# Reordering VectorE, ScalarE and GpSimd in the first and last steps of a dense layer behind attention and experts

## What is computed

```
def _moe_ref(x, w_gate, w1, w2):          # N=3072 tokens, D=512, E=8, F=1024
    ...
        h = np.maximum(xe @ w1[e], 0.0)
        ye = h @ w2[e]
        out[mask] = gate_w[mask, None] * ye

def _moe2_ref(x, w_in, w_out):            # w_in 512 x 2048, w_out 2048 x 512
    h = x @ w_in
    g = h - np.tanh(h)
    return (g @ w_out).astype(np.float32)
```

## Time and profile before

| | us |
|---|---|
| median of 3 runs | 1126.31 (1126.26 to 1127.74) |
| profiled execution, its own time | 1127.19 |
| its span | 1125.4 |
| PE busy | 1090.5 (97%) |
| DVE, ACT, POOL busy | 611.1, 478.8, 491.3 |

### The profile page before, as it was taken

One profiled execution on the slowest core, in us unless ns is written; L12 is line 12 of the kernel. 1 busy time (PEld: TensorE's weight loads), 2 busy tenths in 40 slices (PEclk: granted clock), 3 DMA queues, 4 the chain that ended last, 5 costly groups with the idle time before them and its releaser, 6 DMA issues.

```text
span 1125.4 us, 17079 instructions
## 1 busy us (share of the span) xinstructions
PE 1090.5 (97%) x5993; PEld 870.8 (77%) x5993; DVE 611.1 (54%) x1326; ACT 478.8 (43%) x1016; POOL 491.3 (44%) x494
## 2 busy tenths in 40 slices
PE   8999998799999999999989999999999999999995
PEld 5766765588888888888867888888888888888884
DVE  5787777232223222322258666666666666666664
ACT  6788875324233424351354333333333333333331
POOL 3246625617016345483175335335335335435432
PEclk9999999899999999999999999999999999999998
DMA  7545832534215243464241100001010010000000
GB/s 255 196 129 172 269 108 95 169 121 148 86 57 188 94 159 122 139 217 159 66 132 57 31 17 38 19 20 38 10 29 38 1 38 38 1 1 38 1 1 38
DMA packets 37916, 99.44 MB, mean 88 GB/s; under 512 B 8272, under 2 KB 8400, under 8 KB 32720
## 3 DMA queue, kind: packets, MB, share of 16 engines
q1 hardware_dynamic: 29392, 52.30, 15.0%
q0 software_dynamic: 8448, 46.17, 11.9%
HBM read 75.84 MB, written 22.61 MB: 87 GB/s over the span
## 4 chain that ended last, share of the span: by engine, by line
PE 88%; DVE 5%; POOL 3%; issue 2%; ACT 1%; DMA 1%; POOLq 0%; DVEq 0%; SPq 0%; ACTq 0%
PE bank L676 22%; PE bank L668 21%; PE bank L604 14%; PE bank L618 14%; PE bank L462 4%; PE bank L428 3%; PE bank L444 2%; PE bank L610 2%; DVE prob L932 1%; PE bank L591 1%; POOL weights L1299 1%; PE bank L656 1%; POOL sq L1389 1%; PE bank L504 1%; PE bank L494 1%
## 5 line engine op out<-in xcount | busy, mean ns | idle before, releaser
L1299 POOL TENSOR_TENSOR weights<-raw,weights 128x1024 fp32r<-128x1024 f32 x72 | 171.3, 2399 | 201.7 <-ACT weights L724 201.1
L668 PE MATMUL bank<-mT_hi,weights 128*128 128x512 f32 x768 | 252.2, 390 | 1.7 <-DVE mT_lo L1126 1.7
L676 PE MATMUL bank<-weights,gT_hi 128*128 128x512 f32 x768 | 242.7, 397 | 5.6 <-DVE gT_lo L1183 5.4
L1388 POOL TENSOR_SCALAR ser<-ser 128x512 f32<-128x512 f32 x96 | 63.8, 665 | 286.7 <-DVE ser L1165 286.6
L676 PEld LDWEIGHTS bank<-weights,gT_hi 128*128 128x128 f32 x768 | 142.7, 190 | 39.6 <-DVE gT_lo L1183 11.0
L668 PEld LDWEIGHTS bank<-mT_hi,weights 128*128 128x128 f32 x768 | 144.4, 188 | 32.0 <-DVE mT_lo L1126 2.0
L676 PE MATMUL bank<-weights,gT_lo 128*128 128x512 f32 x384 | 150.9, 393 | 0.0
L604 PE MATMUL bank<-weights,mT_hi 128*128 128x512 f32 x464 | 148.0, 400 | 1.5 <-issue 1.5
L668 PE MATMUL bank<-mT_lo,weights 128*128 128x512 f32 x384 | 149.5, 389 | 0.0
L618 PE MATMUL bank<-weights,hT_hi 128*128 128x512 f32 x464 | 148.7, 401 | 0.0
L875 ACT ACTIVATE bank<-bank 128x512 f32<-128x512 f32 x96 | 55.9, 582 | 213.9 <-DVE ser L1175 213.9
(11 more groups left out here) (141 smaller groups left out, 1577.8 us busy)
## 6 DMA issues: line engine op xcount, KB each, us to landing
raw<-w_all POOLq DMA_DIRECT2D x32, 1024.0 KB, 5.5
raw<-w_all SPq DMA_DIRECT2D x8, 1024.0 KB, 7.0
sorted_y<-ys SPq DMA_DIRECT2D x30, 257.0 KB, 3.3
xs<-sorted_x SPq DMA_DIRECT2D x29, 257.0 KB, 2.8
kT<-kt SPq DMA_DIRECT2D x24, 264.0 KB, 2.8
qT<-qt SPq DMA_DIRECT2D x24, 256.0 KB, 3.2
v_in<-vt SPq DMA_DIRECT2D x24, 256.0 KB, 3.8
raw<-sorted_y SPq DMA_DIRECT2D x20, 257.0 KB, 2.7
```

Of the source, the lines that this page charges most:

```text
L668: done = e.matmul(bank[HB[n % 3]][:, :], wt[:, f // 2, c, cols], x[:, c, :], start=(c == 0 and m == 0), stop=(c == CH - 1 and m == 2))
L676: done = e.matmul(bank[YB[i]][:, :], x[:, n % 3, rows], wt[:, f, :], start=(f == 0 and m == 0), stop=(f == GCH - 1 and m == 2))
L1299: e.tensor_tensor(lo, src, hi.bitcast(F32), ALU.subtract).then_inc(s_w_lo, 1)
L1388: e.tensor_scalar(row, row, SERIES_2, 1.0, ALU.mult, ALU.add).then_inc(s_ser, 1)
```

## The change

- **Last expert.** DVE splits low halves 6 and 7 of `w_in` after its (first) slot, on a new semaphore; GpSimd's steps 1 and 2 lose them, and the fourth load of `w_out` moves ahead of its step 0. PE waits on the new semaphore for these two.
- **First steps.** DVE's low half 0 of `w_out` goes ahead of series(0); the comparison of step 0 goes from GpSimd to DVE; in step 1 curve(0) comes first, then series(1), then g_lo(0). ScalarE's step 1 has square(1) and tanh(1) ahead of g_hi(0).
- **Steps 2 to 94.** DVE's g_lo(n-1) stands at the end of step n, behind low half n-1 of `w_out` where there is one; at the end of a group it now stands ahead of the two copies.
- **Last steps.** In step 95 DVE does curve(94) ahead of series(95), then g_lo(94), then the comparison of step 95. PE runs four more matmuls, whose result nobody reads, between down(94) and down(95).

```
 tensor:
                     if j == 0 and f % 2 == 0:
-                        e.wait_ge(s_w_lo, 8 * W_IN + f // 2 + 1)
+                        if f // 2 < 6:
+                            e.wait_ge(s_w_lo, 8 * W_IN + f // 2 + 1)
+                        else:
+                            e.wait_ge(s_in_lo, f // 2 - 5)
...
+                    if m == STEPS - 1:
+                        e.wait_ge(s_graw, m - 1)
+                        for _ in range(4):
+                            e.matmul(bank[HB[(m - 2) % 3]][:, :], gT_hi[:, (m - 1) % 3, 0:P], woh[:, 0, :],
+                                     start=True, stop=True)
 scalar:
+                if n < STEPS:
+                    square(n)
+                    tanh(n)
                 if n == 1:
                     e.wait_ge(s_row_ids, GROUP)
                     e.wait_ge(y_all, 1)
-                    g_hi(0)
-                    square(1)
-                    tanh(1)
-                else:
-                    if n < STEPS:
-                        square(n)
-                        tanh(n)
-                    if 2 <= n <= STEPS:
-                        g_hi(n - 1)
+                if 1 <= n <= STEPS:
+                    g_hi(n - 1)
 vector, experts:
                 slot_body()
+                if x == E - 1:
+                    for n, y in enumerate((6, 7)):
+                        src, hi, lo = w_half(W_IN, y)
+                        e.wait_ge(s_w_hi, 8 * W_IN + y + 1)
+                        e.tensor_tensor(lo, src, hi.bitcast(F32), ALU.subtract).then_inc(s_in_lo, 1)
 vector, second layer:
+            def small(n):
+                e.wait_ge(s_w, n + 1)
+                u = sq[:, n % 2, :]
+                e.tensor_scalar(u, u, SMALL_U, None, ALU.is_gt).then_inc(s_small_dve, 1)
...
-                if 3 <= n:
-                    g_lo(n - 2)
...
-                if 1 <= n <= 8:
-                    src, hi, lo = w_half(W_OUT, n - 1)
-                    e.wait_ge(s_w_hi, 8 * W_OUT + n)
-                    e.tensor_tensor(lo, src, hi.bitcast(F32), ALU.subtract).then_inc(s_out_lo, 1)
-                if n == 1:
+                if n == 0:
+                    w_out_lo(0)
+                    series(0)
+                    small(0)
+                elif n == 1:
                     curve(0)
+                    series(1)
                     g_lo(0)
-                    series(1)
-                else:
-                    if n < STEPS:
-                        series(n)
-                    if 2 <= n <= STEPS:
-                        curve(n - 1)
+                elif n < STEPS - 1:
+                    series(n)
+                    curve(n - 1)
+                    if n <= 8:
+                        w_out_lo(n - 1)
+                    g_lo(n - 1)
+                elif n == STEPS - 1:
+                    curve(n - 1)
+                    series(n)
+                    g_lo(n - 1)
+                    small(n)
+                elif n == STEPS:
+                    curve(n - 1)
+                    g_lo(n - 1)
 gpsimd:
+            e.wait_ge(s_in_lo, 2)
+            load_raw(W_OUT, 3)
...
-                    e.tensor_scalar(u, u, SMALL_U, None, ALU.is_gt).then_inc(s_small, 1)
-                if n == 1:
-                    split_lo(W_IN, 6)
-                if n == 2:
-                    split_lo(W_IN, 7)
-                    e.wait_ge(s_w_lo, 8 * W_IN + 8)
-                    load_raw(W_OUT, 3)
+                    if 0 < n < STEPS - 1:
+                        e.tensor_scalar(u, u, SMALL_U, None, ALU.is_gt).then_inc(s_small, 1)
```

More of the change, by code:

```diff
@@ L229, in build @@
         s_w_hi, s_w_lo, s_out_lo, s_expert = sem("w_hi"), sem("w_lo"), sem("w_out_lo"), sem("expert_done")
+        s_in_lo = sem("w_in_lo_by_vector")
         x_turned, x_hi, x_split = sem("slot_x_turned"), sem("slot_x_hi"), sem("slot_x_split")
@@ L239, in build @@
         s_up, s_sq, s_w, s_ser, s_small = sem("up"), sem("sq"), sem("series_w"), sem("series"), sem("small")
+        s_small_dve = sem("small_by_vector")
         s_tanh, s_t, s_cp, s_graw, s_ghi, s_glo = (sem("tanh"), sem("t"), sem("t_picked"), sem("g_raw"), sem("g_hi"),
@@ L1166, in series, with w_out_lo @@
                                        in1=sq[:, n % 2, :], op0=ALU.add, op1=ALU.mult).then_inc(s_w, 1)
+            def small(n):
+                e.wait_ge(s_w, n + 1)
+                u = sq[:, n % 2, :]
+                e.tensor_scalar(u, u, SMALL_U, None, ALU.is_gt).then_inc(s_small_dve, 1)
+            def w_out_lo(y):
+                src, hi, lo = w_half(W_OUT, y)
+                e.wait_ge(s_w_hi, 8 * W_OUT + y + 1)
+                e.tensor_tensor(lo, src, hi.bitcast(F32), ALU.subtract).then_inc(s_out_lo, 1)
             def curve(n):
@@ L1173, in curve @@
                 e.wait_ge(s_t, n + 1)
-                e.wait_ge(s_small, n + 1)
+                if n in (0, STEPS - 1):
+                    e.wait_ge(s_small_dve, 1 if n == 0 else 2)
+                else:
+                    e.wait_ge(s_small, n)
                 e.copy_predicated(row, sq[:, n % 2, :].bitcast(I32), bank[MT][:, :]).then_inc(s_cp, 1)
```

## The result

The changed kernel takes 1129.28 us (median of 13 runs, 1128.28 to 1130.07), the kernel before 1126.88 in the same comparisons. The ratio is 1.0025, 95% interval 1.0017 to 1.0032: it is slower by 2.8 us (2.4 by the medians). Forecast were 1123.0 us, some 3 us faster than before, and a range of 1121.3 to 1128.

The account below looks back on a forecast made before the run. PE, busy 97% of the span, was taken as the bound, so only its waits could be won back. 1127.19 - 4.3 + 0.2 + 1.7 - 1.5 = 1123.3 us, carried to the median as 1123.0; range 1121.3 to 1128.

Parts of the forecast that it names:

- Last expert: VectorE's low halves 6 and 7 before step 0: GpSimd gives way early, PE starts 0 to 0.3 us late, priced +0.2.
- rival 1: Before step 0: GpSimd holds VectorE off to its instruction's end, PE 2.6 us late plus half clock; about 1127 us; chance 0.35.
- Rival 2: Before step 0: GpSimd wins twice, half 7 starts at 573.3, PE 5.1 us late; about 1129.5 us; chance 0.1.
- forecast case: Whole kernel: the main forecast of 1123.0 us, own range 1121.3 to 1125, chance 0.48.
- Ends of groups: Five group ends: g_lo ahead of copies costs PE 0.18 us, later stores 0.15 each time; loss 1.7 us, bounds 0.9 to 3.
- First steps: Steps 0 to 5: down(0) at 580.5 and up(6) at 599.8 us, gain 4.3 us, range 3.6 to 4.7.
- rival 3: First steps: VectorE can't keep step time with a low half ahead of g_lo, no gain; 1126 or so; chance 0.07.
- Last steps: Layer's end: PE idles 0.5 us for g_lo(94), not 2.19, and keeps full clock; gain 1.5 us, 1.2 to 2.0.

Follow-up runs that it names:

- GpSimd yields: Changed kernel, but GpSimd starts its low halves 4 and 5 of w_in only when VectorE's two are done: 1126.60 us, ratio 1.0006 to the kernel before.
- the low halves back: Changed kernel, but low halves 6 and 7 of w_in are GpSimd's in steps 1 and 2 again: 1125.54 us, ratio 0.9998 to the kernel before.
- the group ends alone: Kernel before, with only g_lo put ahead of the two copies at the five group ends: 1129.94 us, ratio 1.0035.
- the last steps alone: Kernel before, with only the changed order, VectorE comparison and four extra matmuls of the last steps: 1124.75 us, ratio 0.9986.

## Why the prediction was wrong

**Last expert: the step that failed first.** The price of +0.2 us rested on GpSimd giving way before the last 0.2 us of its low half, as a GpSimd comparison had seemed to. It did not: both of VectorE's low halves ended 1.08 us after GpSimd's did, so all but some 0.14 of their 1.22 us came behind it. The lateness of rival 1 came as described, 2.5 us where it said 2.6. Even its own premise didn't carry the price: with 0.2 us half 6 would have ended at 568.5, when GpSimd's next low half (568.38) had already been asked for; the sum's 568.3 needed GpSimd to give way 0.4 us before its end. I had weighed one row of each kind, and generalised the wrong one: the 2.50 us low half in the earlier trace rows stood beside a GpSimd comparison, the pair here beside GpSimd's two-input subtraction, and the row that showed the same GpSimd instruction (66.66 us in the earlier trace rows) had VectorE held to its end. That VectorE instruction at 67.88 adds a constant and has one input in SBUF; the prediction calls it a comparison. The page "SBUF — State Buffer" of the Trainium skill, section "Who interferes with whom", says that a VectorE instruction with two SBUF inputs contends with a GpSimd one that reads SBUF, for ports under an exclusive lock. The 1.92, 3.37 and 2.87 us rows agree. Why the 2.50 us low half got through before the comparison's end was not tested. Rival 2 did not happen: VectorE, waiting, got its turn between GpSimd's two low halves.

**Clock.** Rival 1 priced the half clock at 1.7 us; up(0) took 5.50 in place of 2.72, and 2.4 us of it reached down(0) (1.8 in the timing). The forecast case had none for it, and even its own 0.3 us of lateness may not have been free: in the run where GpSimd yields, a wait of 2.04 us was followed by half clock.

**Ends of groups: the term that was mis-sized.** It was 2.8 us too low, after the 4.7 of lateness and clock at the start the second largest error. The mechanism was right in both parts; the second was sized far too low. The first copy behind g_lo cost 0.29 us each time (0.18 forecast), the stores another 0.6 (0.15 taken, 0.4 as the upper bound). The sum is 4.5 us in the traces and 3.9 to 4.1 in the timing, against 1.7 forecast and 3 as the bound. What I left out: the delayed comparison also meets VectorE's next series (680.82 us in the changed kernel's trace) and takes 1.96 us, not 1.49, and each wait of TensorE costs some 0.15 us more when the matmuls restart.

**First steps.** Right. With the clock up, down(0) came 15.24 us after the transposes; less the 2.5 of lateness that is 12.7, and 12.71 were measured with the low halves back, where the prediction has 580.5 - 568.0 = 12.5. VectorE kept the step time with the low half ahead of g_lo, so rival 3 fell: down(0) to down(3) took 16.57 us (584.29 to 600.86) for six passes of 2.72, 16.3. A gain of 4.2 was there to be had (4.3 forecast), of which 3.55 also with the low halves left in GpSimd's steps 1 and 2. Which of the new orders in these steps brings it, the earlier low half 0, the comparison on VectorE or g_lo within its own step, was not taken apart.

**Last steps.** Right in its mechanism, 1.85 us in the trace and 1.6 alone against 1.5 forecast. g_lo(94) met GpSimd's scaling and took 1.14 us, and TensorE waited 0.80 us where 0.5 was forecast. The four extra matmuls do nothing.

In all, with the prices from the traces: -4.2 + 2.5 + 2.4 + 4.5 - 1.85 = +3.3, as they show. The -4.2 is what the 0.7 us at down(3) leaves once lateness and clock are taken off, so the sum comes out by its making; the lateness, the clock, the group ends and the last steps were each measured by themselves. Rival 1, the nearest, gave +0.2: it had the lateness, and lacked 2.8 us of the group ends and 0.7 of the clock.

## What to carry to other kernels

An instruction put into an engine's idle time is only free if nothing else holds what it needs: look up what the neighbour does in that stretch, and price it by the row with the same kind of instruction on the neighbour, not by the nearest in size. When two operations swap places, follow what each one releases: here the copies had sat in a wait for another engine at no cost, and moving them behind delayed four stores, a comparison and a pick, two steps on. A cost that recurs per group weighs more than one that comes once, and splitting a change into its parts showed two good ones, the first and the last steps, under two bad.

## What was not expected of the hardware

- A VectorE subtraction of two SBUF tensors, 1.22 us alone, took 1.92 and 3.37 us beside GpSimd's subtractions, and ended 1.08 us after each of them; one that takes 0.69 us alone took 2.87.
- The comparison on VectorE, SBUF to SBUF in 128x512, took 0.43 us (0.69 taken in the prediction), 1.5 us on GpSimd.
- The length of a TensorE wait alone doesn't tell whether half clock follows. Waits of 2.04 us (GpSimd yields), 2.14 and 2.19 (the kernel before) and 4.20 (the changed kernel) were followed by it, waits of 0.80 to 1.74 were not. But nor was the wait of 2.12 us at down(0) in the two runs that start as the kernel before does, the group ends alone and the last steps alone, where the kernel before has 2.14 and then half clock. In the first of the two:

```profile
581.58 0.73 PE L676 MATMUL bank<-weights,gT_hi 128*128 128x512 f32 x2 [2.12 <-DVE gT_lo L1183]
```

  In this trace the granted clock was 1.00 from there to 588 us. down(3) came 33.52 us after the transposes in all three, so there the half clock cost nothing that lasted.
